# A third PSUM bank for turned probabilities, and the first MLP's first x split on POOL: a fused attention + two-MLP kernel

## The reference, cut to what matters

```python
scores = scale * np.matmul(q, k.transpose(0, 1, 3, 2))
cum = np.cumsum(np.maximum(s, 0.0), axis=-1)
bias = -(cum[:, :, :, None] - cum[:, :, None, :])
scores = np.where(causal, -1000000000.0, scores + np.minimum(bias, 0.0))
attn = np.exp(scores - np.max(scores, axis=-1, keepdims=True))
attn = attn / (np.sum(attn, axis=-1, keepdims=True) + 1e-09)
x = heads_to_tokens(np.matmul(attn, v))          # 2304 x 512
h = x @ w_in;  x = (h - np.tanh(h)) @ w_out      # first MLP
h = x @ w2_in; ...softmax, h * sm, layer norm... # second MLP
out = ln @ w2_out
```

## Time and profile before

| what | value |
|---|---|
| median of 3 runs | 839.49 us (839.37 to 840.57) |
| the profiled execution's own time | 839.61 us |
| its span, first to last instruction | 837.8 us |
| PE busy | 815.6 us, 97% of the span |
| DVE, ACT, POOL busy | 448.0, 386.4, 193.3 us |
| mean granted TensorE clock | 0.996 |

### The profile page before, as it was taken

The page is one execution under the profiler, slowest core; times in us unless marked ns, Lnnn a source line. Parts: engine busy times, 40 slices in busy tenths (PEclk is TensorE's granted clock), DMA queues, the critical chain, the costliest instruction groups (busy, mean ns, idle before and its releaser), DMA issues.

```text
span 837.8 us, 14362 instructions
## 1 busy us (share of the span) xinstructions
PE 815.6 (97%) x4552; PEld 706.1 (84%) x4552; DVE 448.0 (53%) x1033; ACT 386.4 (46%) x872; POOL 193.3 (23%) x234
## 2 busy tenths in 40 slices
PE   6999999998999999999999999999999999999998
PEld 5788888876888888888888888899988888888886
DVE  5888988898854342233223322324647554555452
ACT  4998898887544232232223222324523433233323
POOL 3677787784100000000000000000022211221110
PEclk9999999999999999999999999999999999999999
DMA  7564555554343200000000000000200100000001
GB/s 180 141 155 121 152 155 144 129 139 144 96 146 101 76 1 0 1 1 0 0 0 0 0 0 0 0 1 26 76 0 2 38 13 25 25 25 13 25 25 38
DMA packets 77715, 46.30 MB, mean 55 GB/s; under 512 B 59824, under 2 KB 68144, under 8 KB 77680
## 3 DMA queue, kind: packets, MB, share of 16 engines
q1 hardware_dynamic: 75232, 45.19, 19.0%
q10 hardware_dynamic: 2448, 0.66, 0.4%
HBM read 40.97 MB, written 4.87 MB: 55 GB/s over the span
## 4 chain that ended last, share of the span: by engine, by line
PE 89%; DVE 5%; issue 2%; ACT 1%; DVEq 0%; ACTq 0%
PE psum L1202 24%; PE psum L1215 24%; PE psum L1413 12%; PE psum L1441 11%; PE psum L1300 6%; PE psum L1329 4%; PE psum L1257 4%; PE psum L1427 2%; DVE pT_lo L980 2%; PE psum L1275 2%; DVE probs L997 1%; PE psum L1261 1%; PE psum L1345 1%; DVE x_low L1011 1%; DVE x_sum L1020 1%
## 5 line engine op out<-in xcount | busy, mean ns | idle before, releaser
L1202 PE MATMUL psum<-x_hi,w1i 128*128 128x464 f32 (+1 forms) x640 | 185.7, 371 | 0.5 <-DVE w1i L926 0.5
L1215 PE MATMUL psum<-gate_hi,w1o 128*128 128x464 f32 (+1 forms) x640 | 146.5, 371 | 0.0
L1202 PEld LDWEIGHTS psum<-x_hi,w1i 128*128 128x128 f32 x640 | 119.7, 188 | 14.9 <-DVE w1i L926 0.9
L1215 PEld LDWEIGHTS psum<-gate_hi,w1o 128*128 128x128 f32 x640 | 120.1, 188 | 13.6
L960 DVE TENSOR_TENSOR gate_lo<-gate,gate_hi 128x464 fp32r<-128x464 f32 (+1 forms) x80 | 51.1, 639 | 135.8 <-ACT gate_hi L705 135.8
L1202 PE MATMUL psum<-x_lo,w1i 128*128 128x464 f32 (+1 forms) x320 | 118.8, 371 | 0.0
L705 ACT ACTIVATE gate_hi<-gate 128x464 fp32r<-128x464 f32 (+1 forms) x80 | 47.2, 590 | 147.1 <-PE psum L1215 137.8
L950 DVE TENSOR_TENSOR gate<-psum,gate 128x464 f32<-128x464 f32 (+1 forms) x80 | 50.9, 637 | 97.2 <-ACT gate L694 97.2
L619 POOL CAST y_hi<-xT 128x512 fp32r (+1 forms) x18 | 11.0, 613 | 387.6 <-PE psum L1202 384.2
L694 ACT ACTIVATE gate<-psum 128x464 f32<-128x464 f32 (+1 forms) x80 | 44.2, 552 | 107.1 <-PE psum L1202 105.1
L1441 PE MATMUL psum<-w2o,lnT_hi 128*128 128x512 f32 x288 | 91.8, 400 | 0.6 <-DVE lnT_lo L1158 0.6
(11 more groups left out here) (113 smaller groups left out, 1270.7 us busy)
## 6 DMA issues: line engine op xcount, KB each, us to landing
cum_bc<-cum_dram SPq DMA_DIRECT2D x16, 576.0 KB, 4.7
rden_T<-rden_dram SPq DMA_DIRECT2D x32, 144.0 KB, 3.0
out_x<-out_sb SPq DMA_DIRECT2D x18, 256.0 KB, 2.0
stage<-in_q SPq DMA_DIRECT2D x32, 128.0 KB, 2.4
v_raw<-in_v SPq DMA_DIRECT2D x32, 128.0 KB, 3.6
stage<-in_moe_w_in SPq DMA_DIRECT2D x16, 256.0 KB, 2.9
stage<-in_moe_w_out SPq DMA_DIRECT2D x16, 256.0 KB, 3.0
stage<-in_k SPq DMA_DIRECT2D x28, 128.0 KB, 2.3
```

The source lines that it names most:

```text
L1202: mm = pe.matmul(h_ps[j % 4][:, 0:wide(c)], wp[j][:, kt, :], xp[:, kt, 0:wide(c)], start=(n == 0), stop=(n == 3 * KT - 1))
L1215: mm = pe.matmul(y_ps[m][:, 0:wide(c)], wp[j][:, m * P:(m + 1) * P], gp[j % 2][:, 0:wide(c)], start=(j == 0 and wp is w1o_hi and gp is gat ...
```

## The change

Two things. First, unit B2 is turned into bank 5, which holds q and k in transit and is free between slot s's third q/k copy and the next slot's first q/k transpose; B3 takes bank 4. The waits follow: B2 waits for `qk_copied` of the third part (ACT's copy out of bank 5), B3 for `p_lo` of T, the next slot's A01 for B01, and A2 for all seven units of the pair before. Second, the split of x for chunk 0 leaves ACT and DVE and goes to POOL (`first_x` in its `slot`), tiles 0 to 2 in slot 15 behind the splits of q and k (which slot 15 no longer has) and ahead of `scale_x` and `split_v`, tile 3 in slot 16 ahead of `scale_x`.

```diff
-        turn_ps = {"A01": bank(3), "A2": bank(4), "A3": bank(3), "T": bank(4), "B01": bank(3), "B2": bank(4), "B3": bank(3)}
+        turn_ps = {"A01": bank(3), "A2": bank(4), "A3": bank(3), "T": bank(4), "B01": bank(3), "B2": bank(5), "B3": bank(4)}
...
+                def first_x(*tiles):
+
+                    for kt in tiles:
+                        pool.wait_ge(cum_copied, 2 * PAIRS)
+                        wait(pool, x_lo_done, kt)
+                        pool.tensor_copy(x_hi[:, kt, :], xT[:, kt, 0:CH]).then_inc(x_hi_done, 1)
+                        pool.wait_ge(x_hi_done, kt + 1)
+                        pool.tensor_tensor(x_lo[:, kt, :], xT[:, kt, 0:CH], x_hi[:, kt, :].bitcast(F32),
+                                           ALU.subtract).then_inc(x_lo_done, 1)
...
+                if sl.fixed and sl.s == PAIRS - 1:
+                    first_x(0, 1, 2)
+                    pool.wait_ge(x_lo_done, 3)
+                if sl.fixed and sl.s == PAIRS:
+                    first_x(3)
+                    pool.wait_ge(x_lo_done, 4)
                 scale_x()
                 split_v()
...
-                first_x(sl, 3)
-                first_x(sl, 0)
...
                         if unit == "A01":
                             pe.wait_ge(probs_const, 2)
                             pe.wait_ge(exped, TILES * pair + 2)
-                            wait(pe, p_lo_done, UNITS * pair)
+                            wait(pe, p_lo_done, UNITS * (pair - 1) + NTH["B01"])
                         elif unit == "A2":
                             pe.wait_ge(exped, TILES * pair + 5)
+                            wait(pe, p_lo_done, UNITS * pair)
                         else:
                             pe.wait_ge(exped, TILES * pair + (7 if unit == "A3" else TILES))
-                            pe.wait_ge(p_lo_done, UNITS * pair + NTH[unit] - 2)
+                            if unit != "B2":
+                                pe.wait_ge(p_lo_done, UNITS * pair + NTH[{"A3": "A01", "T": "A2", "B01": "A3", "B3": "T"}[unit]])
+                            elif sl.runs(1):
+                                pe.wait_ge(qk_copied, 3 * sl.pair(1)[0] + 3)
```

More of the change, by code:

```diff
@@ L659, in _, with split_x @@
             load_tokens(act, k_raw[1], k_pairs, 1, qk_in[1])
-            def split_x(c, tiles=range(KT)):
+            def split_x(c):
                 wait(act, up_done, FT * c)
-                for kt in tiles:
+                for kt in range(KT):
                     act.activation(x_hi[:, kt, 0:wide(c)], xT[:, kt, tokens(c)], ACT.Copy).then_inc(x_hi_done, 1)
@@ L707, in step @@
                     w1i_hi_part(j + AHEAD - 1)
[L710 to L713, removed]
             def first_w1i(sl, j):
@@ L805, in slot @@
                 qk_copy(2)
-                first_x(sl, 1)
                 exp(1, 2)
@@ L810, in slot @@
                 first_w1i(sl, 2)
-                first_x(sl, 2)
                 p_hi("B2")
@@ L963, in step @@
                     w1i_lo_part(j + AHEAD - 1)
-            def first_x(sl, kt):
-                if sl.fixed and sl.s == (PAIRS if kt == KT - 1 else PAIRS - 1):
-                    split_x(0, (kt,))
             def first_w1i(sl, j):
```

## The result

| | before | after |
|---|---|---|
| median of the runs (6 each, side by side) | 840.10 us (839.37 to 841.40) | 835.14 us (833.82 to 835.89) |
| the profiled execution's own time | 839.61 us | 835.15 us |
| its span | 837.8 us | 833.3 us |
| PE busy | 815.6 us | 816.6 us |

The ratio of the medians is 0.9937, 95% interval 0.9924 to 0.9950. 833.4 us were forecast. 835.1 lies inside the range of 831.1 to 837.0, but outside the forecast's own 832.0 to 834.8, and 4.5 us came instead of 6.2 between the two profiled executions.

A forecast was written before the change was run, and what follows sets the result against it. The prediction took a closed ring of DVE and PE work, with B2 in PE's part, to bound the loop. 3.8 - 0.2 + 2.8 - 0.2 = 6.2 us off 839.61 gave 833.4 us, range 831.1 to 837.0.

The forecast's parts named there:

- What bounds: Loop slots: a closed ring of about 7.3 us of DVE and about 5 us of PE, with B2 in PE's part.
- B2 out of the ring: Loop, slots 2 to 14: B2's own run of 0.31 us leaves each slot's ring, 3.8 us gained in all.
- POOL's pace of 12.3: Loop: POOL's own round exceeds the new 12.08 us slots; it falls 2.1 us back, 1.9 covered by slack, 0.2 charged.
- loop slots of 12.3 us: Sign that the prediction is wrong; if right, loop slots would last 12.0 to 12.1 us.
- POOL paces the loop at once: Rival, loop: a consumer with less slack is held, so the loop gains 0.8 for 2.8; 835.4 us, chance 0.14.
- Slots 15 and 16: Splitting x on POOL instead of DVE and ACT brings `first_up(0)` from 211.62 to 208.8: 2.8 us gained, 0.2 charged.
- the rival on the clock: PE's clock still falls in slot 15, a stretch there staying up to 1.4 us longer: 834.8 us, chance 0.08.
- The charge of 0.3 for `den`: Slot 15: DVE's `den` slows from 0.16 to 0.46 us beside busy POOL, leaving 0.3 of 0.6 us gained.
- POOL's margin: Slots 15 and 16: x's splits on POOL finish just when `first_up(0)` needs them; 0.2 us charged.
- debt: POOL's lateness carried from the loop into slot 15, taken as 1.9 us.
- DVE's subtraction of the first weights: Slot 16: beside POOL work it could end about 0.3 us after PE asks for it, making the sum 833.7.
- its band of no change: Whole kernel: changes within about 0.2%, 1.7 us, count as same; chance 0.07.

The follow-up runs named there:

- e3: Changed kernel with the addition of 1e-9 to the denominators (`den`) left out, reciprocal taken straight from the row sums: 834.63 us, ratio 0.9920 to the kernel before.
- e7: Kernel before the change, with the addition of 1e-9 to the denominators (`den`) left out: 837.13 us, ratio 0.9961 to the kernel before.
- e4: Changed kernel with POOL's two `cum_tail` copies cut from 576 to 64 columns for all pairs but the first: 831.22 us, ratio 0.9890 to the kernel before.
- e5: Changed kernel with the tail's bias loaded by two transfers on SP's queue instead of copied by POOL: 845.94 us, ratio 1.0062 to the kernel before.

## Why the prediction was right, and which term was off

**What bounds.** Right: a ring of DVE's row from PE's first scores to `p_lo` of T, and PE's from there on. Shown by e3 and e7, where DVE lost one instruction, and by e4, where that instruction lost its block: the slots followed.

**B2 out of the ring.** Right, and to size: PE's part from `p_lo` of T to the next first scores went from 3.59 us (125.85 to 129.44) to 3.31 (125.30 to 128.61), 0.28 against the 0.31 worked out from the earlier trace rows. A wait of about 0.1 stays at `attend`, as the prediction had it.

**What failed: DVE's part was taken as fixed.** It was 8.82 us from the slot's first scores (117.03 to 125.85) and became 8.99 (116.31 to 125.30); the 0.17 is `den`, 0.46 before and 0.64 after. The prediction had that row in hand and read it as a price that POOL's work puts on `den`, charged only in slot 15. In fact it ended with POOL's second copy there (121.30 and 121.28), this row of the kernel before's POOL timeline:

```profile
120.61 0.67 POOL L542 COPY cum_tail<-cum_bc 64x576 f32<-64x576 f32 x1 [0.17 <-POOL cum_tail L539]
```

`den` ends with the copy it meets, so it is a meeting point: from slot 6 on the loop ran no faster than POOL, with 1.29 us of the semaphores' slack left. POOL's pace of 12.3 was forecast, and charged 0.2 us because the readers of its results had 2.28 us to spare. That slack was there (e3 used it up). The loop gained 2.48 us and not 3.6, and loop slots of 12.3 us, one of the prediction's signs of being wrong, came true.

The Trainium skill, "SBUF — State Buffer", section "Who interferes with whom", counts `tensor_scalar` among the DVE operations that can take the port pair shared with POOL, and says that the later one then stands for the whole instruction; the trace agrees (0.64 for 0.16 us, over with the copy). I had weighed that section's line on two SBUF inputs and passed this one by.

**The rival "POOL paces the loop at once"** gave 835.4 us, nearest to what was measured. Its effect came, from slot 6 on, but by none of the consumers it thought of: not a wait on a semaphore, which the list of waits would have shown. That its total is so near is partly luck: it left slots 2 to 14 a gain of 1.6 us (3.6 less 2.0) and they gave 2.48, slots 15 and 16 gave 0.6 more than forecast, and the later start took 1.3 in the profile.

**Slots 15 and 16.** Mechanism right, a little more than forecast: 3.22 for 2.8 - 0.2. The clock stayed at 1.00, so the rival on the clock is out. The charge of 0.3 for `den` was not due (0.16 at 194.12), nor the 0.2 for POOL's margin: POOL's second copy of slot 15 ended 4.82 us into the slot, for 3.88 before, so POOL came with 0.9 us of debt and not 1.9, since the loop had kept its pace. POOL's last `x_lo`, at 205.78, met DVE's subtraction of the first weights, as the prediction had thought possible:

```profile
205.79 0.68 DVE L933 TENSOR_TENSOR w1i<-stage,w1i 128x512 fp32r<-128x512 f32 x1
```

There POOL paid, 1.73 us for 1.19, though its row begins 0.01 us ahead; by the rule of the Trainium skill ("SBUF — State Buffer", "Who interferes with whom"), which blocks the later one, it should have been DVE. Rows 0.01 us apart may not tell which came first. PE waited for neither.

**The sum.** 6.2 - 1.1 (loop) + 0.6 (slots 15 and 16) = 5.7; the profiled execution then lost 1.3 in slot 1 to a wait for k and the clock behind it, and shows 4.4 at `first_up(0)`. The medians of the runs side by side differ by 5.0. One sum of the prediction is off: POOL's pace with the clock and an `x_hi` late by 1 us comes to 837.8 (835.4 + 1.4 + 1.0) and not 838.2, which is still at the edge of its band of no change.

## What to carry to other kernels

Before a wait is removed, look at every short instruction in the loop whose time differs between slots: if it ends when an instruction on another engine ends, the two engines are tied there, and the slower one's round is the next bound, though no list of waits names it. Two edits that shorten the same ring need not add: the third bank and the missing `den` gave 2.4 and 3.8 us in the loop, and together 3.8, since POOL's pace is the next bound for both. In a loop whose queues are all nearly full (in slot 9 PE is busy 12.1 us of 12.3, DVE 11.3, ACT 11.1, and POOL's row has no wait for another engine), work taken from the slowest pays only on the queue with room at that moment: here ACT (2.6 us less in the loop, not yet seen in the whole time), not DVE (1.8 more), and not SP, whose row of issues is busy time that the page of the profile doesn't count.

## What the runs showed that I had not expected

- A TENSOR_SCALAR on 9 columns took 0.64 us, four times its 0.16, with the whole of POOL's COPY; the RECIPROCAL right behind it took 0.20 to 0.22 beside the second copy.
- An issue of SP takes some 0.35 to 0.76 us in the loop (one of e5 took 1.97), and two more a slot, with a ninth of the bytes, made slots 2 to 14 3.0 us longer.
- PE's list of waits was all but empty in the loop while PE came to `attend` 0.41 us a slot later than in e4; the offset of an instruction within its slot, compared with a faster kernel, showed it.
